# A float32 convolution and FFN kernel on one core: the first piece is convolved by two engines and turned by TensorE, weight remainders are made by chunks, and a narrow piece is closed before the next begins

## The reference, cut to what matters

```python
# x (4, 4096, 192), weight_gen (4, 4096, 8 heads, 7 taps), w_in (192, 2048), w_out (2048, 192), float32
w = exp(weight_gen - max over the 7 taps)
w = w / (sum over the 7 taps + 1e-9)
out[b, s, head, c] = sum over k of w[b, s, head, k] * x_pad[b, s + k, head, c]   # 24 channels a head
h = out.reshape(16384, 192) @ w_in
g = h * sigmoid(1.702 * h)
result = g @ w_out
```

## Time and profile before

| | us |
|---|---|
| median of 3 runs (lowest to highest) | 1134.61 (1134.56 to 1135.12) |
| the profiled execution | 1135.54 |
| its span, first to last instruction | 1133.7 |
| PE busy in the span | 1107.6 (98%) |
| DVE busy | 812.1 (72%) |
| ACT busy | 620.6 (55%) |
| first matmul starts | 20.65 |

### The profile page before, as it was taken

How to read it: one execution, slowest core, us unless ns; L and a number is a source line. 1 busy time by engine, 2 the same in 40 slices (tenths; PEclk the granted TensorE clock), 3 DMA queues, 4 the chain that set the end, 5 groups by cost and what they waited for, 6 DMA issues and landing times.

```text
span 1133.7 us, 21631 instructions
## 1 busy us (share of the span) xinstructions
PE 1107.6 (98%) x9728; PEld 916.2 (81%) x9728; DVE 812.1 (72%) x709; ACT 620.6 (55%) x653; POOL 0.2 (0%) x4
## 2 busy tenths in 40 slices
PE   2999999999999999999999999999999999999998
PEld 2888788888888888888888888888888888888886
DVE  8898978769486684957859487594866849578322
ACT  5777665464554645546464554645546455454543
POOL 0000000000000000000000000000000000000000
PEclk9999999999999999999999999999999999999999
DMA  7501010100201010010100101002010100100000
GB/s 246 183 15 52 16 40 15 40 29 1 67 1 40 29 38 30 1 39 29 39 29 1 44 25 39 29 1 67 1 39 29 38 29 1 40 28 2 28 1 29
DMA packets 8348, 41.23 MB, mean 36 GB/s; under 512 B 1024, under 2 KB 1152, under 8 KB 5952
## 3 DMA queue, kind: packets, MB, share of 16 engines
q1 hardware_dynamic: 8256, 39.85, 10.8%
HBM read 24.12 MB, written 12.58 MB: 32 GB/s over the span
## 4 chain that ended last, share of the span: by engine, by line
PE 95%; DVE 3%; ACT 1%; issue 1%; DMA 0%; ACTq 0%; DVEq 0%
PE hid L441 45%; PE acc_main L459 30%; PE acc_rest L459 20%; DVE prod L314 1%; DVE conv L321 1%; ACT gate L252 0%; DVE conv L314 0%; DVE gate_lo L406 0%; DMA taps<-in_tap_runs 0%; ACT gate_hi L255 0%; ACT xt L225 0%; ACT xt L216 0%; ACT xt L220 0%; ACT L210 0%; DVE prod L339 0%
## 5 line engine op out<-in xcount | busy, mean ns | idle before, releaser
L252 ACT ACTIVATE gate<-hid 128x1024 f32<-128x1024 f32 x256 | 263.0, 1027 | 482.4 <-PE hid L441 482.2
L406 DVE TENSOR_TENSOR gate_lo<-gate,gate_hi 128x1024 fp32r<-128x1024 f32 x256 | 311.9, 1219 | 254.9 <-ACT gate_hi L255 254.1
L441 PE MATMUL hid<-xt,w_hi 64*128 64x512 f32 x3072 | 433.8, 388 | 20.7 <-ACT xt L235 20.6
L441 PEld LDWEIGHTS hid<-xt,w_hi 64*128 64x128 f32 x3072 | 289.9, 185 | 81.0 <-ACT xt L216 20.6
L459 PE MATMUL acc_main<-gate_hi,w 64*128 64x512 f32 x2048 | 316.0, 386 | 0.4 <-DVE outs_main L381 0.4
L255 ACT ACTIVATE gate_hi<-hid 128x1024 fp32r<-128x1024 f32 x256 | 261.2, 1020 | 0.0
L459 PEld LDWEIGHTS acc_main<-gate_hi,w 64*128 64x128 f32 x2048 | 192.3, 184 | 40.7 <-issue 1.1
L441 PE MATMUL hid<-xt,w_lo 64*128 64x512 f32 x1536 | 217.0, 388 | 0.0
L459 PE MATMUL acc_rest<-gate_hi,w 64*128 64x512 f32 x1024 | 200.0, 387 | 0.0
L459 PE MATMUL acc_main<-gate_lo,w 64*128 64x512 f32 x1024 | 199.8, 386 | 0.0
L459 PE MATMUL acc_rest<-gate_lo,w 64*128 64x512 f32 x1024 | 199.7, 386 | 0.0
(11 more groups left out here) (28 smaller groups left out, 197.5 us busy)
## 6 DMA issues: line engine op xcount, KB each, us to landing
xwin<-in_x_runs SPq DMA_DIRECT2D x15, 1056.0 KB, 5.0
out<-outs_main SPq DMA_DIRECT2D x13, 512.0 KB, 2.7
out<-outs_rest SPq DMA_DIRECT2D x13, 256.0 KB, 2.9
taps<-in_tap_runs SPq DMA_DIRECT2D x1, 3136.0 KB, 15.5
taps<-in_w_rows SPq DMA_DIRECT2D x2, 1536.0 KB, 9.2
w_hi<-w_hi SPq DMA_DIRECT2D x2, 768.0 KB, 8.2
w_lo<-w_lo SPq DMA_DIRECT2D x2, 768.0 KB, 7.2
out<-outs_main SPq DMA_DIRECT2D x6, 256.0 KB, 2.1
```

The costliest lines, as they stand in the source:

```text
L252: nc.scalar.activation(gate[:, v % 2, :, :], hid[:, v % 2, :, :], ACT.Gelu_apprx_sigmoid).then_inc(gate_ready, 1)
L406: nc.vector.tensor_tensor(gate_lo[:, v % SLOTS, :, :], gate[:, v % 2, :, :], gate_hi[:, v % SLOTS, :, :], ALU.subtract).then_inc(gate_lo_r ...
L441: last = nc.tensor.matmul(hid[:, v % 2, h, :], w[rows, k, q, f], xt[rows, j % 2, part, k, :], start=(i == 0), stop=(i == len(terms) - 1))
```

## The change

Piece 0 is prepared in another way. Its 8 tokens lie as 4 tokens on each partition with all 192 channels (new inputs `x_first`, `tap_first`), the products and sums keep the shape 128x768. GpSimd makes the products of 3 of the 7 taps and one sum, DVE the other 4 products and the sums. DVE's accumulator and the taps that it uses lie in PSUM. The last sum is split into three slices; TensorE turns each with four 128x128 transposes against an identity (a new input), after four warm-up matmuls on plain float32 data. ACT and DVE copy the turned slices to the high part, DVE subtracts slice by slice.

ACT rounds w2 in two parts. DVE makes the low parts of the weights in smaller chunks: first what the first units need, the rest behind `gate_lo` of units 1, 3 (w1) and 2, 4, 5 (w2) of piece 0. SP's taps for pieces 4 to 17 now wait for the last of these.

Around the ends of pieces 0 to 3 PE's order becomes second(j-1,6), second(j-1,7), first(j,0), first(j,1), first(j,2), second(j,0); `lift` and `evict` of these pieces move from unit 1 to unit 0. The tables of steps and of the rounding change.

```diff
-STEPS_AT = ((0, 6, 3, 3, 3, 3, 5, 3),
-            (2, 1, 3, 2, 3, 5, 4, 4),
-            (1, 0, 4, 1, 5, 2, 2, 2),
-            (1, 0, 1, 2, 2, 2, 1, 0),
+STEPS_AT = ((0, 4, 2, 3, 2, 3, 3, 2),
+            (2, 2, 3, 3, 3, 3, 3, 3),
+            (1, 2, 3, 2, 3, 5, 1, 2),
+            (1, 1, 2, 2, 2, 2, 2, 4),
             (0, 0, 0, 5, 2, 1, 2, 1, 2, 2, 1, 2, 0, 1, 0, 0))
-ROUND_AT = (6, 5, 4, 6, 12)
+ROUND_AT = (7, 7, 7, 7, 12)
+WARM_UP = 4
+SHARED = 3
...
+        def closes_first(j):
+            return 1 <= j <= len(NARROWS)
...
-            sp.wait_ge(w1_lo_ready, 2)
+            sp.wait_ge(w1_lo_ready, 5)
...
-            sp.wait_ge(w2_lo_ready, 2)
+            sp.wait_ge(w2_lo_ready, 8)
             load_taps(4, LAST, taps_loaded[2])
...
-            nc.scalar.activation(w2[:, :, 0:D], w2_raw, ACT.Copy).then_inc(w2_hi_ready, 1)
-            round_piece(0)
-            nc.scalar.activation(other(0, LOWER, 0), turned(0)[UPPER], ACT.Copy).then_inc(hi_crossed, 1)
-            cross_remainders(0)
+            nc.scalar.activation(w2_of(0, 2, slice(0, D)), w2_of(0, 2, slice(0, D), w2_raw), ACT.Copy
+                                 ).then_inc(w2_hi_ready, 1)
+            act.wait_ge(head_summed, 1)
+            nc.scalar.activation(head_conv[:, :, SLICES, :], head_conv[:, :, 0, :], ACT.Copy).then_inc(head_again, 1)
+            for k in (0, 2):
+                act.wait_ge(head_turned_ready, k + 1)
+                nc.scalar.activation(xt[:, 0, 0, k, :], head_turned[k], ACT.Copy).then_inc(head_hi_act, 1)
+            nc.scalar.activation(w2_of(2, CH // 2, slice(0, D)), w2_of(2, CH // 2, slice(0, D), w2_raw), ACT.Copy
...
+                    if v == 0 and closes_first(j):
+                        lift(j - 1)
...
-            maxima_and_shift(0)
-            for q in range(CONV_STEPS):
-                conv_step(dve, 0, q)
-            turn_piece(0)
...
+                dve.wait_ge(head_op, 4)
+                dve.wait_ge(x_loaded, 16)
+                mul(0, head_acc)
+                mul(1, head_prod[0])
+                mul(2, head_prod[1])
...
+                add(head_prod[0])
...
+                mul(3, head_prod[0])
+                add(head_prod[1])
...
+                add(head_prod[0])
...
+                dve.wait_ge(shared_op, 1)
+                add(shared_prod[0])
...
+                dve.wait_ge(shared_op, SHARED + 1)
+                for k in range(SLICES):
...
+                    nc.vector.tensor_tensor(head_conv[:, :, k, :].rearrange("p u (a c) -> p u a c", a=2), a, b, ALU.add
+                                            ).then_inc(head_summed, 1)
...
+            w1_remainder(slice(0, P))
+            dve.wait_ge(head_turned_ready, 2)
+            nc.vector.tensor_copy(xt[:, 0, 0, 1, :], head_turned[1]).then_inc(head_hi_dve, 1)
...
+            w1_remainder(slice(P, 2 * P))
+            w1_remainder(slice(2 * P, 4 * P))
+            w2_remainder(0, 2)
...
-                    if v == EVICT_AT and j > 0:
+                    if j > 0 and v == (0 if closes_first(j) else EVICT_AT):
                         evict(j - 1)
...
+                    if j == 0 and v in (1, 3):
+                        w1_remainder(slice((v + 3) * P, (v + 5) * P))
+                    if j == 0 and v in (2, 4, 5):
+                        done = {2: 2, 4: 4, 5: 6}[v]
+                        w2_remainder(done, done + 2)
...
+            for i in range(SHARED):
+                k = ALONE + i
+                nc.gpsimd.tensor_tensor(shared_prod[i].rearrange("p (g c) -> p g c", c=GRP),
...
+            pool.wait_ge(shared_op, SHARED)
+            nc.gpsimd.tensor_tensor(shared_prod[2], shared_prod[1], shared_prod[2], ALU.add).then_inc(shared_op, 1)
...
+                for i in range(WARM_UP):
+                    nc.tensor.matmul(hid[:, 0, 0, :], flat[:, i * P:(i + 1) * P], flat[:, N:2 * N], start=True, stop=True)
...
+                    for u in range(FIRST):
+                        two = head_conv[:, u, k:k + 2, :].rearrange("p k c -> p (k c)")
+                        last = nc.tensor.transpose(head_turned[k][:, u * P:(u + 1) * P], two, ident[:])
+                    last.then_inc(head_turned_ready, 1)
...
+            turn_head()
             for j in range(LAST + 1):
+                if closes_first(j):
+                    for v in range(UNITS[j - 1] - LAG, UNITS[j - 1]):
+                        second_product(j - 1, v)
                 for v in range(UNITS[j]):
                     first_product(j, v)
                     if v >= LAG:
                         second_product(j, v - LAG)
-                    elif j > 0:
+                    elif j > 0 and not closes_first(j):
                         second_product(j - 1, v - LAG + UNITS[j - 1])
```

More of the change, by code:

```diff
@@ L91, in ffn_of_dynamic_conv @@
         outs_rest = sb("outs_rest", [HALF, 2, N])
+        x_head = gate[:].rearrange("p b h n -> p (b h n)")[:, 0:FIRST_WIN * D].rearrange("p (t d) -> p t d", d=D)
+        head_prod = [prod[:, k, 0:N_FIRST] for k in range(2)]
+        shared_prod = [prod[:, 0, N_FIRST:N_CONV], prod[:, 1, N_FIRST:N_CONV], conv[:, 0:N_FIRST]]
+        head_flat = outs_main[:].rearrange("p h n -> p (h n)")
+        head_conv = head_flat.rearrange("p (u k c) -> p u k c", k=SLICES + 1, c=HALF)
         hid = ctx.enter_context(nc.psum_tensor("hid", [P, 2, 2, N], F32))
@@ L129, in kind, with w2_of, slice_of @@
             return min(j, len(NARROWS))
+        def closes_first(j):
+            return 1 <= j <= len(NARROWS)
+        def w2_of(first, last, cols, of=w2):
+            return of[:].rearrange("p (q c) d -> p q c d", q=2)[:, :, first:last, cols]
+        def slice_of(h, k):
+            return (k + h) % SLICES
+        MAIN, MAIN_LO = slice(0, P), slice(2 * P, 3 * P)
+        REST_COLS, REST_HI, REST_LO = slice(P, 2 * P), slice(P, D), slice(D, 2 * P)
         def tap_span(first, last):
@@ L218, in cross_rounded @@
             def cross_rounded(j):
-                for there, here in ((LOWER, UPPER), (UPPER, LOWER)):
+                for there, here in ((LOWER, UPPER), (UPPER, LOWER))[0:1 if j == 1 else 2]:
                     nc.scalar.activation(other(j, there, 0), turned(j)[here], ACT.Copy).then_inc(hi_crossed, 1)
             def cross_remainders(j):
-                act.wait_ge(xt_lo_ready, j + 1)
+                act.wait_ge(xt_lo_ready, j)
                 for there, here in ((LOWER, UPPER), (UPPER, LOWER)):
@@ L256, in _ @@
                                          ).then_inc(gate_hi_ready, 1)
-                    if v == EVICT_AT and j > 0:
+                    if v == EVICT_AT and j > 0 and not closes_first(j):
                         lift(j - 1)
@@ L343, in split_piece @@
             def split_piece(j):
-                dve.wait_ge(xt_hi_ready, j + 1)
+                dve.wait_ge(xt_hi_ready, j)
+                if j == 1:
+                    nc.vector.tensor_copy(other(j, UPPER, 0), own(j, 0)[LOWER].bitcast(F32)).then_inc(hi_crossed, 1)
                 nc.vector.tensor_tensor(own(j, 1), turned(j), own(j, 0), ALU.subtract).then_inc(xt_lo_ready, 1)
@@ new lines, in _ @@
+            head()
+            dve.wait_ge(w1_hi_ready, 1)
+            w1_remainder(slice(0, P))
+            dve.wait_ge(head_turned_ready, 2)
+            nc.vector.tensor_copy(xt[:, 0, 0, 1, :], head_turned[1]).then_inc(head_hi_dve, 1)
+            for k in range(SLICES):
+                if k == 1:
+                    dve.wait_ge(head_hi_dve, 1)
+                else:
+                    dve.wait_ge(head_hi_act, 1 + k // 2)
+                nc.vector.tensor_tensor(xt[:, 0, 1, k, :], head_turned[k], xt[:, 0, 0, k, :], ALU.subtract
+                                        ).then_inc(head_lo, 1)
@@ L386, in evict @@
                 if is_narrow(j):
-                    halves = ((slice(0, HALF_N), slice(HALF_N, N)), (slice(HALF_N, N), slice(0, HALF_N)))
+                    fore, aft = slice(0, HALF_N), slice(HALF_N, N)
+                    halves = ((fore, aft), (aft, fore)) if j else ((fore, fore), (aft, aft))
                     dve.wait_ge(main_out_act, j + 1)
@@ L516 @@
         "tap_runs": wg.reshape(2, LANES, run, 2, hb * k).transpose(0, 3, 1, 2, 4).reshape(P, run * hb * k),
+        "x_first": _np.stack([windows[:, s * head:s * head + head + k - 1] for s in range(2)], axis=1
+                             ).reshape(P, head + k - 1, d),
+        "tap_first": wg.reshape(runs, run, h * k)[:, 0:NARROW].reshape(P, head * h * k),
+        "identity": _np.eye(P, dtype=x.dtype),
         "w1_rows": w_in.reshape(2, SLICES, 32, 2, f // 2).transpose(3, 0, 2, 1, 4).reshape(P, SLICES, f // 2),
@@ L531 @@
     for u in PIECES:
-        cols = pieces[:, 2 * LANES * at:2 * LANES * (at + u)].reshape(d, 2, u, LANES)
-        out[:, :, at:at + u] = cols.transpose(1, 3, 2, 0)
+        cols = pieces[:, 2 * LANES * at:2 * LANES * (at + u)]
+        if at:
+            out[:, :, at:at + u] = cols.reshape(d, 2, u, LANES).transpose(1, 3, 2, 0)
+        else:
```

(1 more changed line is left out.)

145 lines of the change are left out of this document (105 added, 40 removed).

## The result

| | before | after |
|---|---|---|
| median, us (lowest to highest) | 1134.59 (1134.53 to 1135.12), 4 runs | 1144.78 (1144.53 to 1145.87), 4 runs |
| the profiled execution | 1135.54 | 1144.86 |
| its span | 1133.7 | 1143.0 |
| mean granted clock of PE | 1.000 | 0.996 |

The ratio is 1.0091, its 95% interval 1.0073 to 1.0108: the change makes the kernel 10.2 us slower. The forecast was 4.8 us slower. The sign, the places of the waits and the gain of the head came out as worked out; the size did not, and the time lies 0.3 us above the range.

What follows compares the result with a forecast made beforehand. PE was taken as the bound (95% of the chain): boundary waits 13.25 in place of 2.36 lose 10.9, the head wins 6.1, net +4.8 us. Forecast 1139.4 us; 8-in-10 range 1133.5 to 1144.5.

Steps and rivals of the forecast that it cites:

- What bounds the kernel: Whole kernel: PE is 95% of the chain; only its start (20.65), 2.99 lost early and 2.36 at boundaries can be won.
- The head: Before the first second-product: it starts at 23.7 instead of 29.76, gaining 6.1 us; bounds 4.5 and 7.
- Piece 0 and its end: DVE's added remainders in piece 0 make PE wait 1.6, 0.4, 1.1 and 0.9: 4.0 us at this boundary.
- End of piece 1: Split(2) waits for ACT's rounding behind unit 7, so gate_lo of unit 7 is late and PE waits 0.3 us.
- End of piece 2 and ahead of piece 4: Split(3) stands before its rounding, DVE idles some 4 us, PE waits 2.6; DVE overfull in piece 3 costs 6.35.
- the boundary terms 2.6 and 6.35: PE's forecast waits in us: 2.6 at the end of piece 2, 6.35 at the end of piece 3.
- the clock as a rival of 0.17: Clock falls in the 4.45 us gap before piece 4: 1142.4 us, chance 0.17.
- the 2.99 taken from the earlier trace: Us lost before the first second-product in the kernel before, to the low clock after 20 us of PE idling.
- The sum: Boundaries 13.25 in place of 2.36, so 10.9 lost; head 6.1 won; net +4.8 us, forecast 1139.4.
- The other side: Rival: piece 4 turned by F+43.9 (F: end of first(2,7)) instead of F+48.2; 1126.2, or 1132 with half the waits; chance 0.11.
- What costs nothing: Taps leave some 15 us later, yet they, the piece 2 window behind them and the weight chunks arrive in time.

Runs made afterwards that it cites:

- Experiment 3: The changed kernel with 24 useless matmuls in PE's gap at the end of piece 2 and 36 ahead of piece 4: 1142.18 us, ratio 1.0064 to before.
- experiment 10: The changed kernel with respread step tables, roundings at units 7, 6, 5, 7, and DVE making one low-part copy of piece 1: 1130.28 us, ratio 0.9962 to before.
- the old loop: Order and step tables of the kernel before, here run with the new head and chunked remainders of the change: 1135.42 us, ratio 1.0007 to before.
- experiments 7 and 8: Late weight remainders moved from DVE to GpSimd, in the changed kernel (1145.14 us) and in the new head with the order and tables of before (1134.3 us).
- experiment 1: The changed kernel with the order and tables of before, its new head and chunked remainders kept: 1135.42 us, ratio 1.0007 to before.
- experiment 6: The changed kernel with mended step tables but PE's old order at narrow piece ends, lift and evict back in unit 1: 1157.27 us, ratio 1.0198 to before.
- experiment 4: The changed kernel without its four warm-up matmuls (WARM_UP 4 to 0): 1146.72 us, ratio 1.0102 to before.

## Why the prediction was right and wrong

- **What bounds the kernel**: right. PE's pace from piece 4 on is unchanged (from first(4,3) to first(17,15) 947.47 us, before 947.46), and the change acts only through PE's start and its waits up to 181 us.
- **The head**: right in mechanism, 0.95 short (7.05 instead of 6.1). x came 0.4 earlier than forecast, GpSimd was inside its 1.86 and not late, and a transpose took 0.11 to 0.13 where 0.2 was taken. The upper bound that the prediction gave, 7 with 0.11 a transpose, is what happened. The estimate by the Trainium skill, page GPSIMD Engine Reference, section Performance versus the Vector engine, was 1.66 plus dispatch; the trace has 1.50 for a product, less than that, and 1.83 for the sum.
- **Piece 0 and its end**: the places and releasers are right, the total of 4.2 instead of 4.0 is partly luck. The waits were 1.23, 0.16, 0.92 and 0.58, where 1.6, 0.4, 1.1 and 0.9 were forecast: 2.9 instead of 4.0. The other 1.3 are matmuls that start slower behind each of the waits (0.2 to 0.4 each), which the forecast didn't have; why they do stays open.
- **End of piece 1**: 1.0 instead of 0.3. The wait for `gate_lo` was the 0.34 forecast; the rest is that PE's first matmuls behind the wait take some 0.2 more, and that another 0.5 are lost up to second(2,0) in small steps without a bracket. At one of them first(2,2), with the second products gone from between, waits a little for `gate_hi` (which ends at 94.59; first(2,2) starts at 94.64). Such small losses were left out of the sum; they make up most of what the terms for the ends of pieces 2 and 3 were short of (0.6 and 0.4).
- **End of piece 2 and ahead of piece 4**: place, releaser and DVE's idling right (3.97 us before split(3), 4 forecast). **Here is the step that failed: the boundary terms 2.6 and 6.35 were priced at full clock.** They measured 4.9 and 8.5, and behind either gap 1.71 were lost in matmuls at the low clock. The prediction had the clock as a rival of 0.17, on the argument that the only low stretch in the trace stood behind 20 us of idling "and no shorter gap is in the trace". That there is no such row said nothing either way. It also looked only at the gap ahead of piece 4, and missed the wait of 2.62 us, behind which the clock fell as well. Even with that rival the time would have been 1142.4, since it priced one gap and no slow starts. Per gap the price was lower than the 2.99 taken from the earlier trace rows. Experiment 3 takes the clock's part away with the waits left in place: the median falls by 2.6, PE's losses by 2.8, of the 3.4. The "1.0" that the prediction read for the granted clock in the first matmuls is no measurement: the trace of before has a clock record only from 26.77 on, which is where the slow pairs end.
- **The sum**: 4.8 forecast, less 0.95 in the head, plus 3.4 in the slow stretches behind the two gaps (2.8 of it shown to be the clock by experiment 3), 0.7 at the end of piece 1, 0.2 at that of piece 0, and 0.6 and 0.4 at the last two: 9.2, as the spans say.
- **The other side**: its condition was that DVE had piece 4 turned by F+43.9. The tables of experiment 10 make DVE early enough (0.4 us lost there), with 11 steps in piece 3 instead of 16 and more in pieces 0 and 1; with the tables of the change it was out of reach, as the count said.
- **"What costs nothing"**, the late taps: right for this kernel. Not for the old loop, where DVE stood 2.04 for the window behind them.

## What to carry to other kernels

When two engines run in written orders, add up the table: up to which unit has the count reached the step that waits for the other engine, and where in that engine's order does the step stand? One entry that is a unit early stops an engine for microseconds and everything written behind it, and can be found on paper. Price a gap of the TensorE twice, once for the wait and once for the clock behind it: in these runs the low clock came behind waits of 1.87 us and more, though not behind each, and cost 1.2 to 1.7 where the wait was 2.62 or 4.28. If it can't be removed, useless matmuls in it can give the second part back. And work taken out of a prologue is only gained if the engine that gets it has room in the next stage: here 4.4 us of it, with the transfer that had to wait for it, ate the gain of a head that was 7 us shorter. A second engine didn't help, since DVE's subtractions took up to 3.4 times as long beside it.

## What was unexpected of the hardware

- The low clock after short waits. By the brackets in PE's rows it came behind waits of 1.87 (experiments 7 and 8), 2.62 and 4.28 (after) and 2.73 (experiment 1), and not behind 1.53 (experiment 1) or 1.69 (after). Two waits of 2.32 in experiment 6 went one each way: behind the one before 92.67 the granted clock was 1.00 over 4 us, behind the one before 130.14 it was 0.61. So the length of the wait alone doesn't decide it here.
- What it costs is not fixed either: in experiment 4, whose wait at the end of piece 2 was the same (2.63), the slow matmuls lasted from 125.23 to 131.37, 6.1 us, where after has 3.75. That may be why such kernels' times spread (1146.15 to 1148.45 there); it wasn't tested. The trace is of the slowest of these runs.
- Four float32 matmuls of 512 columns, given as warm-up, fill 5.6 us and show as eight rows.
- DVE and GpSimd on float32 data in SBUF: a DVE subtraction of 512 columns 3.4 times as long (684 to 2325 ns), a GpSimd one of 768 columns 2.3 to 2.8 us.
